# A convolution and two MLPs in one kernel: the prologue rebuilt, with TensorE summing the first tap products

## What is computed

```python
def _attn_ref(x, weight_gen) -> np.ndarray:
...
    w = weight_gen - np.max(weight_gen, axis=-1, keepdims=True)
    w = np.exp(w)
    w = w / (np.sum(w, axis=-1, keepdims=True) + 1e-09)
    pad = K - 1
    x_pad = np.concatenate([np.zeros((B, pad, D), dtype=np.float32), x], axis=1)
    idx = np.arange(S)[:, None] + np.arange(K)[None, :]
    x_unf = x_pad[:, idx, :]
    x_unf = x_unf.reshape(B, S, K, H, group)
    out = np.einsum('bshk,bskhg->bshg', w, x_unf)
...
    h = np.maximum(x @ w_in, 0.0)
    return (h * h @ w_out).astype(np.float32)
...
    h = x @ w_in
    relu6 = np.clip(h + 3.0, 0.0, 6.0)
    g = h * relu6 / 6.0
    return (g @ w_out).astype(np.float32)
```

## Time and profile before

| | us |
|---|---|
| median of 3 runs | 1168.07 (1165.64 to 1168.88) |
| the profiled execution | 1168.12 |
| its span | 1166.3 |
| TensorE busy | 1153.4 (99%) |
| VectorE busy | 924.5 (79%) |
| ScalarE busy | 675.9 (58%) |

### The profile page before, as it was taken

The page is one execution under the profiler, slowest core; times in us unless marked ns, Lnnn a source line. Parts: engine busy times, 40 slices in busy tenths (PEclk is TensorE's granted clock), DMA queues, the critical chain, the costliest instruction groups (busy, mean ns, idle before and its releaser), DMA issues.

```text
span 1166.3 us, 26723 instructions
## 1 busy us (share of the span) xinstructions
PE 1153.4 (99%) x10412; PEld 1147.6 (98%) x10412; DVE 924.5 (79%) x1054; ACT 675.9 (58%) x772; POOL 3.7 (0%) x11
## 2 busy tenths in 40 slices
PE   7999999999999999999999999999999999999998
PEld 7999999999999999999999999999999999999997
DVE  8889797887968879697786978879688796976565
ACT  6887645556555565645556455564555556555554
POOL 1000000000000000000000000000000000000000
PEclk9999999999999999999999999999999999999999
DMA  7211003020030200202011020200302002010001
GB/s 214 79 63 53 5 2 76 4 66 12 0 74 4 70 9 13 61 4 72 6 49 29 0 74 4 65 14 0 74 4 69 10 13 61 0 38 3 1 15 28
DMA packets 78190, 41.93 MB, mean 36 GB/s; under 512 B 55952, under 2 KB 72462, under 8 KB 78156
## 3 DMA queue, kind: packets, MB, share of 16 engines
q1 hardware_dynamic: 78156, 41.45, 13.8%
HBM read 30.00 MB, written 11.40 MB: 36 GB/s over the span
## 4 chain that ended last, share of the span: by engine, by line
PE 94%; ACT 2%; DVE 1%; DMA 1%; issue 1%; SPq 0%; DVEq 0%; ACTq 0%
PE h_ps L910 45%; PE y_ps L921 30%; PE y_ps L930 20%; DMA stage<-in_moe_w_in_dram 1%; ACT hid L444 1%; ACT hid L449 1%; ACT win L431 0%; ACT hid_hi L457 0%; DVE acc L610 0%; DVE hid_lo L711 0%; SPq L292 0%; DVE prod L632 0%; DVE wout L677 0%; DVE hid L700 0%; SPq L302 0%
## 5 line engine op out<-in xcount | busy, mean ns | idle before, releaser
L910 PE MATMUL h_ps<-xt,win 64*128 64x512 f32 (+1 forms) x4860 | 1068.9, 379 | 1.0 <-DVE wout L677 0.9
L910 PEld LDWEIGHTS h_ps<-xt,win 64*128 64x128 f32 x4860 | 826.6, 184 | 2.0 <-DVE wout L677 1.3
L921 PE MATMUL y_ps<-hid_hi,wout 64*128 64x512 f32 (+1 forms) x2160 | 562.5, 379 | 0.7 <-DVE win L677 0.5
L460 ACT ACTIVATE hid_hi<-hid 128x1024 fp32r<-128x1024 f32 (+1 forms) x244 | 256.4, 1051 | 316.8 <-DVE hid L702 155.5
L711 DVE TENSOR_TENSOR hid_lo<-hid,hid_hi 128x1024 fp32r<-128x1024 f32 (+1 forms) x270 | 313.2, 1160 | 143.0 <-ACT hid_hi L460 137.8
L921 PEld LDWEIGHTS y_ps<-hid_hi,wout 64*128 64x128 f32 x2160 | 385.2, 184 | 1.9 <-DVE win L677 0.7
L921 PE MATMUL y_ps<-hid_lo,wout 64*128 64x512 f32 (+1 forms) x1080 | 323.1, 378 | 1.0 <-DVE hid_lo L711 1.0
L930 PE MATMUL y_ps<-hid_lo,wout 64*128 64x512 f32 (+1 forms) x1080 | 322.9, 378 | 0.0
L930 PE MATMUL y_ps<-hid_hi,wout 64*128 64x512 f32 (+1 forms) x1080 | 322.8, 378 | 0.0
L921 PEld LDWEIGHTS y_ps<-hid_lo,wout 64*128 64x128 f32 x1080 | 194.6, 184 | 1.7 <-DVE hid_lo L711 1.4
L930 PEld LDWEIGHTS y_ps<-hid_hi,wout 64*128 64x128 f32 x1080 | 194.6, 184 | 0.2
(11 more groups left out here) (87 smaller groups left out, 325.8 us busy)
## 6 DMA issues: line engine op xcount, KB each, us to landing
xwin<-in_x_dram SPq DMA_DIRECT2D x14, 960.0 KB
by_feature<-stage SPq DMA_DIRECT2D x52, 96.0 KB, 2.0
out_dram<-outs SPq DMA_DIRECT2D x240, 16.0 KB, 1.5
out_dram<-outs SPq DMA_DIRECT2D x240, 8.0 KB, 1.4
stage<-by_feature SPq DMA_DIRECT2D x13, 256.0 KB, 3.0
stage<-in_moe_w_out_dram SPq DMA_DIRECT2D x8, 384.0 KB, 5.8
stage<-in_moe_w_in_dram SPq DMA_DIRECT2D x4, 512.0 KB, 6.9
stage<-in_moe_w_in_dram SPq DMA_DIRECT2D x8, 256.0 KB, 6.2
```

The source lines that it names most:

```text
L460: act.activation(hi, hid[:, slot, :, 0:width], ACT.Copy).then_inc(hi_done, 1)
L910: return pe.matmul(h_ps[:, s % 2, t, 0:tokens.stop - tokens.start], win[layer][r, wn, cols], src[r, xn, tokens], start=bool(rows) and n in ...
L921: return pe.matmul(ps[:, 0, tokens], wout[layer][r, tile, w_cols], src, start=bool(rows) and s == 0 and n == 0, stop=not rows and s == STE ...
```

## The change

The steady loop stays as it is, but for the softmax: its weights get an eighth column that holds the small constant 1e-9, set once by POOL, so that the row sum takes it in and the separate addition (L668) goes. In the prologue:

- **Taps of chunk 0.** VectorE only multiplies (`tap_products`); the adds go. Each of the seven products goes to TensorE by itself, whose transposes add up in PSUM (`turn_product`, 8 transposes each). Half 0 is turned so at once, with one identity matmul behind each product and three more at the end; half 1 in step 7 (four products) and at the head of step 8 (three). Taps are taken from the last to the first, and six buffers hold products.
- **Halo.** It is loaded in a near part (the three rows next to the tokens) and a far part, four loads each instead of four in all.
- **Weights.** w_in comes in quarters (512 columns) instead of halves; 12 pieces a layer instead of 8, a ring of 6 buffers instead of 5. The high parts of w_out pieces 4, 7 and 10 of layer 1 are VectorE's (`weight_hi`, a copy of 128x768), and their low parts, like those of the pieces beside them, stand one or two steps later or earlier than before.
- **Steps 0 and 1 together.** `first_sums` does the four tiles' first products, then their second, then their third; 20 matmuls as before.
- **POOL** makes the identity matrix first and zeroes the halo's edge after it; ten identity matmuls stand ahead of the first turn.
- **Chunk 1** reads a window in the same wide buffer, loaded with rows 4 to 7 behind piece 10; the window of chunk 2 is then loaded without a wait for chunk 1.

```diff
-    PC = FF // 2
+    QC = FF // 4
     PT = 4
-    STAGES = 5
-
-
-    PIECE = [("in", 0, 0), ("in", 0, 1), ("out", 0, 0), ("in", 1, 0), ("in", 1, 1)]
-    PIECE += [("out", n, 0) for n in range(1, FT // PT)]
+    STAGES = 6
+
+
+    PIECE = [("in", 0, 0), ("in", 0, 1), ("in", 1, 0), ("in", 1, 1), ("out", 0, 0), ("in", 2, 0), ("in", 2, 1),
+             ("out", 1, 0), ("in", 3, 0), ("in", 3, 1), ("out", 2, 0), ("out", 3, 0)]
     PIECES = len(PIECE)
 
+    OWN_HI = (4, 7, 10)
+    IN_PART = [1 + PIECE.index(("in", q, 1)) for q in range(4)]
+    OUT_PART = [1 + PIECE.index(("out", n, 0)) for n in range(FT // PT)]
...
-    WARM = 26
+    WARM = 10
...
+        probs_of = prob[:, :].rearrange("p (n k) -> p n k", k=SLOTS)
+        products = [buf[:, n * JHALF * D:(n + 1) * JHALF * D] for buf in (acc, prod[:, 0, :], prod[:, 1, :]) for n in range(2)]
...
             load_gates(0)
-            load_first_half()
-            for n in range(3):
+            load_rows(0, JHALF, x_own_loaded)
+            load_halo(HALO // 2, HALO // 2, x_near_loaded)
+            load_halo(0, HALO // 2, x_far_loaded)
+            for n in range(5):
                 load_piece(n)
-            load_second_half()
+            load_rows(JHALF, JHALF, x_late_loaded)
+            for n in range(5, PIECES - 1):
+                load_piece(n)
             sp.wait_ge(exp_done, 1)
             load_gates(1)
-            for n in range(3, STAGES):
-                load_piece(n)
-            load_second_window()
-            for n in range(STAGES, PIECES + STAGES):
+            load_rows(J, J, x_second_loaded)
+            for n in range(PIECES - 1, PIECES + STAGES):
                 load_piece(n)
             sp.wait_ge(exp_done, 2)
             load_gates(2)
             load_window(2)
-            for n in range(PIECES + STAGES, 2 * PIECES):
+            for n in range(PIECES + STAGES, 2 * PIECES - 1):
                 load_piece(n)
             sp.wait_ge(exp_done, 3)
             load_gates(3)
+            load_piece(2 * PIECES - 1)
...
-            for n in range(3):
-                split_piece(n)
+            split_piece(0)
+            split_piece(1)
             split_x1_hi(0, xt[1], y1_ps, 0)
+            split_piece(2)
             split_piece(3)
...
-                if g == 6:
+                if g == 7:
                     split_x1_hi(0, xt[1], y1_ps, 1)
...
-                if g in (0, 1, 3, 5):
-                    split_piece((0, 1, 3, 5).index(g) + 4)
+                if g in (1, 3):
+                    split_piece(g // 2 * 3 + 5)
+                    split_piece(g // 2 * 3 + 6)
+                if g == 6:
+                    split_piece(PIECES - 1)
                 if g == 7:
                     exponentials(1)
                 if g == 21:
                     exponentials(2)
-                if g in (8, 10, 24, 26, 28, 31):
-                    split_piece(PIECES + (8, 10, 24, 26, 28, 31).index(g))
+                if g in (8, 9, 10, 11, 24, 26, 28, 30):
+                    split_piece(PIECES + (8, 9, 10, 11, 24, 26, 28, 30).index(g))
...
+            def tap_products(half, ms):
+
+                probs = probs_of[:, half * JHALF * HEADS:(half + 1) * JHALF * HEADS, :]
+                for m in ms:
+                    tap, n = TAPS - 1 - m, half * TAPS + m
+                    if m == 0:
+                        dve.wait_ge(prep_done, prep_value(0, "norm"))
+                        dve.wait_ge(x_late_loaded if half else x_own_loaded, 16)
+                    if n == 1:
+                        dve.wait_ge(x_near_loaded, 32 * B)
+                        dve.wait_ge(halo_zeroed, B)
+                    if n == 1 + HALO // 2:
+                        dve.wait_ge(x_far_loaded, 32 * B)
+                    if n - len(products) == TAPS - 1:
+                        dve.wait_ge(att_turned, 1)
+                    elif n >= len(products):
+                        old = n - len(products)
+                        dve.wait_ge(product_turned, old + 1 - old // TAPS)
+                    src = xwin_first[:, (tap + half * JHALF) * D:(tap + half * JHALF + JHALF) * D]
+                    done(dve.tensor_tensor(products[n % len(products)].rearrange("p (n g) -> p n g", g=GROUP),
+                                           src.rearrange("p (n g) -> p n g", g=GROUP),
+                                           probs[:, :, tap:tap + 1].broadcast_to([P, JHALF * HEADS, GROUP]), ALU.mult))
...
+            def weight_hi(n):
+                hi, raw, loads = piece(n)
+                dve.wait_ge(piece_loaded[n], 16 * len(loads))
+                dve.tensor_copy(hi, raw).then_inc(own_hi, 1)
...
-            taps(0, range(TAPS), 0)
+            tap_products(0, range(TAPS))
             weight_lo(0)
             weight_lo(1)
             split_x1_lo(0, xt[1], y1_ps, 0)
-            for n in range(2, 5):
-                weight_lo(n)
-            taps(0, range(3), 1)
+            weight_lo(2)
+            weight_lo(3)
+            weight_hi(4)
+            weight_lo(4)
             for g in range(HALVES):
                 if g in GATED:
                     gate(g, 0, g % 2, HALF)
-                if g == 1:
+                if g == 2:
                     weight_lo(5)
                     weight_lo(6)
-                if g == 2:
-                    taps(0, [3], 1)
+                    tap_products(1, [0])
+                if g == 3:
+                    weight_hi(7)
                     weight_lo(7)
-                if g in (3, 4):
-                    taps(0, [g + 1], 1)
-                    weight_lo(g + 5)
-                if g == 5:
+                if g == 4:
+                    weight_lo(8)
+                    weight_lo(9)
+                    weight_hi(10)
                     weight_lo(10)
-                    taps(0, [6], 1)
-                if g == 6:
-                    split_x1_lo(0, xt[1], y1_ps, 1)
+                if g in (5, 6):
+                    tap_products(1, range(3 * g - 14, 3 * g - 11))
                 if g == 7:
                     weight_lo(11)
+                    split_x1_lo(0, xt[1], y1_ps, 1)
...
+            def first_sums(src):
+
+                def sums(n):
+                    return h_ps[:, n // PAIR, n % PAIR, 0:HALF]
+
+                tiles = [slice(n * P, (n + 1) * P) for n in range(LAG * PAIR)]
                 pe.wait_ge(x1_hi, 1)
-                for t in range(PAIR):
-                    pe.matmul(sums[t], win[0][:, 0, tiles[t]], src[:, 0, 0:HALF], start=True, stop=False)
-                    pe.matmul(sums[t], win[0][:, 1, tiles[t]], src[:, 0, 0:HALF], start=False, stop=False)
+                pe.wait_ge(piece_lo, 1)
+                for n, tile in enumerate(tiles):
+                    pe.matmul(sums(n), win[0][:, 0, tile], src[:, 0, 0:HALF], start=True, stop=False)
+                    pe.matmul(sums(n), win[0][:, 1, tile], src[:, 0, 0:HALF], start=False, stop=False)
                 pe.wait_ge(x1_lo, 1)
-                for t in range(PAIR):
-                    pe.matmul(sums[t], win[0][:, 0, tiles[t]], src[:, 1, 0:HALF], start=False, stop=False)
+                for n, tile in enumerate(tiles):
+                    pe.matmul(sums(n), win[0][:, 0, tile], src[:, 1, 0:HALF], start=False, stop=False)
                 pe.wait_ge(x1_lo, 2)
                 pe.wait_ge(x1_dup, 1)
-                for t in range(PAIR):
-                    pe.matmul(sums[t], win[0][:, 2, tiles[t]], src[:, 2, 0:HALF], start=False, stop=False)
-                    ins = pe.matmul(sums[t], win[0][:, 3, tiles[t]], src[:, 2, 0:HALF], start=False, stop=True)
-                ins.then_inc(mm1_done, 1)
+                pe.wait_ge(piece_lo, IN_PART[0])
+                for n, tile in enumerate(tiles):
+                    pe.matmul(sums(n), win[0][:, 2, tile], src[:, 2, 0:HALF], start=False, stop=False)
+                    ins = pe.matmul(sums(n), win[0][:, 3, tile], src[:, 2, 0:HALF], start=False, stop=True)
+                    if n % PAIR == PAIR - 1:
+                        ins.then_inc(mm1_done, 1)
+
+            def identities(count):
+                for n in range(count):
+                    pe.matmul(h_ps[:, 0, 0, 0:P], ident[:, :], ident[:, :], start=True, stop=True)
+
+            def turn_product(half, m):
+
+                src = products[(half * TAPS + m) % len(products)]
+                pe.wait_ge(prep_done, prep_value(0, f"mul{m}", half))
+                for j in range(JHALF):
+                    for part in range(2):
+                        col = part * HALF + (half * JHALF + j) * REST
+                        for bank, r in enumerate(ROWS_OF):
+                            ins = pe.matmul(y1_ps[:, bank, col:col + REST], src[r, j * D + part * REST:j * D + part * REST + P],
+                                            ident[r, r], start=m == 0 and j == 0 and part == 0, stop=m == TAPS - 1,
+                                            is_transpose=True, skip_group_check=True, tile_position=(r.start, 0))
```

(21 more changed lines are left out.)

182 lines of the change are left out of this document (84 added, 98 removed).

## The result

The changed kernel takes 1141.99 us (median of 4 runs, 1140.14 to 1142.51), the kernel before 1168.34 in the same comparison (1165.64 to 1168.88). The ratio is 0.9771 [0.9760, 0.9783].

A forecast was written before the change was run, and what follows sets the result against it. The prediction took TensorE, always busy in the steady loop, as the bound, so only its prologue stalls counted: -3.9 - 0.2 + 2.1 - 1.6 + 2.9 = -0.7, from 1168.12 to 1167.4 us, range 1164.7 to 1170.7.

The forecast's parts named there:

- In the steady loop TensorE is busy all of the time: Steady loop: TensorE never stalls, so only the shift of its last stalled prologue step, taken at step 8, moves the end.
- -0.7: Whole prologue up to the second half of step 8: sum of all terms, -0.7 us, giving 1167.4.
- rival A: Prologue start: clock still at the lower level when the sums begin, doubling turns and fillers; +2.95, 1171.1; chance 0.16.
- The prediction's own signs: Prologue: sums at 10.7, step 8's second half at 36.0; wrong if sums start after 12 or either wait is under 1.
- Sums at 10.75, -3.9: Prologue start: first sums begin at 10.75 instead of 14.66, with ScalarE's piece 1 and split last; -3.9 us.
- with one identity matmul of 0.22 it is 0.49 a product: Turns of chunk 0's first half: turn 0.27 plus identity matmul, 0.49 us a product, the pace of VectorE.
- Steps 0 to 3, -0.2: From sums to step 3's second half: 7.35 instead of 7.56, hidden_lo wait gone, piece 4 added, copy taken at 0.94.
- Step 4, a wait of 2.0: Second half of step 4: TensorE idles 2.0 for w_out piece 7, made by VectorE behind hidden_lo 2; +2.1 us.
- Steps 5 and 6, -1.6: Steps 5 and 6: waits for low parts go, 2 x 2.27 instead of 6.11; -1.6 us.
- Steps 7 and 8, a wait of 2.5: Steps 7 and 8: seven turns add 1.9, TensorE idles 2.5 for x1's splits; 9.05 against 6.13, +2.9 us.
- Rivals B and D: Rivals: B, loads later, +0.8, 1168.9, chance 0.12; D, waits at steps 4 and 8 don't show, -5.3, 1162.8, chance 0.03.
- C: Rival, prologue: piece 1 at 9.1, copies at 0.5, both new waits 0.5 shorter; -2.5, 1165.6; chance 0.14.

The follow-up runs named there:

- experiments 2 to 4: Kernel before with the softmax part alone (1139.7), without the small addition (1168.28) or with unused floats (32: 1139.48; 16: 1168.47; 96: 1138.83); changed kernel with 32 floats (1170.56 us).
- experiment 3: The changed kernel with 32 unused floats behind the weights' buffer, against the kernel before: 1170.56 us against 1168.27, ratio 1.0017, trip 70.93.
- experiment 6: Changed kernel with sixteen opening matmuls instead of ten: 1142.39 us; with both moves of experiment 5 and no identity matmul behind each first-chunk turn: 1136.05 us.
- experiment 5: Changed kernel with w_out piece 7 made ahead of hidden chunk 2's low part: 1138.94 us; all half 1 turns at step 7's head: 1138.99; both moves: 1137.3.

## Why the prediction was wrong, step by step

**"In the steady loop TensorE is busy all of the time; so a change to the prologue moves the end only by what it moves TensorE's last stalled step."** This step failed, and it carries all of the 26 us. It went from "never waits" to "takes a fixed time". The pitch of a busy engine was taken as a constant of the instructions; the runs of experiments 2 to 4 show it to depend on where the buffers behind the weights start, their moving operands among them: 68.91 or 70.93 us a trip. The change moved the operands by 1920 bytes, as a side effect of two sizes in its allocations (a stage of 6 x 768 floats for one of 5 x 1024, and 32 floats more of `prob`), and by luck onto a multiple of 256 bytes. Both sizes stand in the diff. Nothing in the trace of before told that its loop was slow, and none of the four rivals was about the loop.

With that set aside (experiment 3) the prologue is to be compared with -0.7, and it is about +2.3. That the 1170.56 of experiment 3 stands near rival A's 1171.1 is luck. The prediction's own signs told it: the sums started after 12, and the second half of step 8 came at 39.65 in the changed kernel, 2.9 later than before. By the same marks as in the working the steps made -2.1, -0.9, +2.2, -0.05 and +3.7, where the forecast had -3.9, -0.2, +2.1, -1.6 and +2.9:

- **Sums at 10.75, -3.9.** Measured 12.58, -2.1. Halo and products were as forecast, and piece 1 was 0.3 late (it reached ScalarE at 10.00, 9.7 had been taken). The term that failed is "with one identity matmul of 0.22 it is 0.49 a product": both durations came from rows where like follows like, and alternating the two added 0.32 (experiment 6). Seven times that is 2.2, which made TensorE the late one instead of ScalarE. Without the fillers (experiment 6) the sums came at 11.24: 1.3 of the 1.8 missed was TensorE's, and the 0.5 left is in the loads and ScalarE's splits, which that run waits for.
- **Steps 0 to 3, -0.2.** From the sums to the second half of step 3 (19.24) it took 6.7, not 7.35: -0.9. The copy of 128x768 took 0.55, not 0.94. This is a row of it:

```profile
22.06 0.55 DVE L698 CAST wout<-stage 128x768 fp32r<-128x768 f32 x1
```

  The row that I took it to be nearest to was the wrong one. Some 0.4 of the 0.7 us can be the copy's; where the rest came from is not shown. The rule cited from the Trainium skill, VectorE: DVE Perf Modes, section "Mode 2×_2P — use both read ports for one tensor", was nearer: 0.4 by its estimate.
- **Step 4, a wait of 2.0.** 1.91: right, with its place and its cause. The clock behind it was missing: 24 to 27 at 0.50, worth 1.6. From the second half of step 4 (23.73) to the turns of step 7 (31.08) it took 7.35, where the working has 5.65.
- **Steps 5 and 6, -1.6.** No wait there, as forecast. The gain was eaten by the clock: to the second half of step 6 (29.79) it took 6.06, before 6.11.
- **Steps 7 and 8, a wait of 2.5.** 2.23, right in place and cause; again the lower level behind it, worth 1.0 up to the second half of step 8. The second half of step 8 came at 39.65, forecast 36.0, before 36.72.
- **Rival A** put the clock's fall at the start, among the turns. It did not fall there. The rule cited for it (the Trainium skill, TensorE: Matmul & The Clock Gate, section "Part 4: PE-mode transpose") would have had it low at the sums; here a string of turns from 6.25 to 9.31 with hardly anything else was followed by sums at the upper level (experiment 6). That is no proof against the rule, since plain matmuls stood ahead of the string and three of them (six records) behind it. The fall came where the working itself had put two idle stretches of 2 us and more, and priced each at its own length. By its length and the lower level behind it the wait of 1.9 costs 3.5 here and that of 2.2 at least 3.2. What taking them out gave is less: 2.8 and 2.9 by the marks in experiment 5, 4.7 for both.
- **Rivals B and D** did not come to pass: the loads were within 0.3 us of their places, and both waits showed. Of **C** only the short copy came, and the waits were not shorter by 0.5.

The statement that ScalarE's and VectorE's savings in the loop are worth nothing held: the kernel without the small addition took 1168.28.

## What to carry to other kernels

A stretch with an engine at 100% is not a stretch of fixed time: before a change is credited or blamed, take the distance of one mark that stands once in each trip, before and after, and if it moved while the loop's instructions did not, look at what the allocations shifted. A pad of a few floats ahead of the matmuls' operands is an experiment of one line, and worth trying on a kernel bound by TensorE (here 28.8 us of 1168). And price an idle TensorE at its length and the slow stretch behind it, and a filler matmul at what it costs among its neighbours, not among its like.

## What the runs showed of the hardware that was not expected

- The pitch of TensorE's paired 64-row matmuls depends on where the buffers behind the weights start in SBUF, the moving operands among them. 70.93 us a trip with `xt`, `hid_hi` and `hid_lo` at 128, 192 or 384 bytes behind a multiple of 512 (70.64 in one trace), 68.91 at 0 or 256, with clock 1.00 and no wait in either: 2.9%. Moving `xt` alone gave 0.42 us a trip, moving `hid_hi` and what follows alone 0.75, of 2.02; which of the buffers make the whole is not shown.
- The slow placement has a second pitch: in one trace two trips of 70.65 and 70.68 were followed by ten of 70.93, after one added matmul of 64 columns on the upper rows. Another trace with 70.64 throughout took 1164.21 us, and three of 13 executions of the kernel before took as long (1164.1 to 1164.7).
- After idle stretches of 1.91 and 2.23 us that began with a busy TensorE at clock 1.00, the clock was 0.50 for some 3 us. It did not always follow: with sixteen opening matmuls, and in the changed kernel with the added matmul, the same wait of 1.91 was followed by 1.00. Nor does it take so long a wait: in the kernel with `hid_hi` moved the longest wait was 0.8 and the clock 0.68 from 15 to 18. In the old prologue this differs from one execution to the next: of twelve traces with it five stay at 1.00 from 15 to 30, like the profiled execution of before, and seven do not.
- An alternation of one 128-row matmul (two records, 0.23 when such follow one another) and one turn of eight 64-row records (0.25 when such follow one another) takes 0.81: 0.33 more, of which at most 0.1 is the turn's mode and target (experiment 6).
- A VectorE copy of 128x768 floats took 0.55, where the subtraction of the same data in two instructions took 1.03.
